# Three edits to one routed attention-MoE-FFN kernel: splits of the open expert's second matrix go from VectorE to GpSimd, early routing moves by a few steps, and the loads of the FFN weights and one scatter change their place

## The reference

```python
# attention: q, k, v are [4, 8, 768, 64]; 4 sink keys and a causal window of 128
scores = (q @ k.T) / sqrt(64), kept where key < 4 or 0 <= query - key < 128
a = softmax(scores); attn_out = a @ v
x = attn_out as [3072 tokens, 512]
# routed experts: top 1 of 8, D = 512, F = 1024
logits = x @ w_gate + modality_bias[modality_id]
e = argmax(logits); gate_w = softmax(logits)[e]
out[t] = gate_w * (relu(x[t] @ w1[e]) @ w2[e])
# FFN: 512 -> 2048 -> 512
h = out @ w_in; g = h * sigmoid(1.702 * h); result = g @ w_out
```

## Time and profile before

| | us |
|---|---|
| median of 3 runs | 1104.38 |
| profiled execution, time | 1103.77 |
| its span | 1102.0 |
| TensorE busy | 1090.4 |
| VectorE busy | 434.9 |
| ScalarE busy | 385.5 |
| GpSimd busy | 347.3 |

### The profile page before, as it was taken

The page is one execution under the profiler, slowest core; times in us unless marked ns, Lnnn a source line. Parts: engine busy times, 40 slices in busy tenths (PEclk is TensorE's granted clock), DMA queues, the critical chain, the costliest instruction groups (busy, mean ns, idle before and its releaser), DMA issues.

```text
span 1102.0 us, 18596 instructions
## 1 busy us (share of the span) xinstructions
PE 1090.4 (99%) x5883; PEld 932.3 (85%) x5884; DVE 434.9 (39%) x1112; ACT 385.5 (35%) x798; POOL 347.3 (32%) x484
## 2 busy tenths in 40 slices
PE   9999999999999999999999999999999999999998
PEld 9999999988888888888888888888888888888887
DVE  5666666679321234122364223222323222222222
ACT  3666667754222133222353222222222222222222
POOL 8899999852466212121120001001001001000100
PEclk9999999999999999999999999999999999999999
DMA  9998899415731133121041001001000001000101
GB/s 217 234 257 202 226 233 245 128 49 181 265 126 38 57 106 132 38 84 40 29 181 58 20 1 48 20 8 42 25 10 38 19 19 38 0 0 0 39 1 39
DMA packets 59700, 96.27 MB, mean 87 GB/s; under 512 B 8192, under 2 KB 33024, under 8 KB 59648
## 3 DMA queue, kind: packets, MB, share of 16 engines
q1 hardware_dynamic: 53888, 76.75, 25.0%
q0 software_dynamic: 5760, 18.89, 5.0%
HBM read 76.21 MB, written 19.41 MB: 87 GB/s over the span
## 4 chain that ended last, share of the span: by engine, by line
PE 94%; DVE 2%; issue 2%; ACT 2%; DVEq 0%; POOL 0%; ACTq 0%; POOLq 0%
PE psum L1264 8%; PE psum L1262 8%; PE psum L1263 8%; PE psum L1255 8%; PE psum L1254 8%; PE psum L1253 8%; PE psum L968 5%; PE psum L1193 4%; PE psum L1162 4%; PE psum L1199 4%; PE psum L1196 4%; PE psum L1166 4%; PE psum L1170 4%; PE psum L943 3%; PE psum L1181 2%; PE psum L931 2%
## 5 line engine op out<-in xcount | busy, mean ns | idle before, releaser
L2048 DVE TENSOR_TENSOR g<-psum,g 128x512 f32<-128x512 f32 x96 | 66.3, 691 | 292.2 <-ACT g L1483 292.2
L1483 ACT ACTIVATE g<-psum 128x512 f32<-128x512 f32 x96 | 57.3, 598 | 305.4 <-PE psum L1255 304.6
L1262 PE MATMUL psum<-w_hi,gT_hi 128*128 128x512 f32 x384 | 151.4, 394 | 0.0
L900 POOL DMA_INDIRECT out<-o_out,out_rows x20 | 21.5, 1074 | 409.3 <-ACT o_out L1503 404.7
L1264 PE MATMUL psum<-w_hi,gT_lo 128*128 128x512 f32 x384 | 149.6, 390 | 0.0
L1263 PE MATMUL psum<-w_lo,gT_hi 128*128 128x512 f32 x384 | 149.6, 390 | 0.0
L1255 PE MATMUL psum<-x2T,win_lo 128*128 (+1 forms) x384 | 149.6, 389 | 0.0
L1253 PE MATMUL psum<-x2T,win_hi 128*128 (+1 forms) x384 | 149.6, 389 | 0.0
L1254 PE MATMUL psum<-x2T,win_hi 128*128 (+1 forms) x384 | 149.4, 389 | 0.0
L968 PE MATMUL psum<-v_sb,pT 128*128 128x73 f32 x704 | 106.2, 270 | 3.2 <-DVE pT L1773 1.6
L1761 DVE CUSTOM_DVE_ANT_0 s_msk<-psum,mask_sb 128x260 f32<-128x260 f32 (+1 forms) x192 | 75.1, 403 | 68.8 <-PE psum L932 37.6
(11 more groups left out here) (313 smaller groups left out, 1884.9 us busy)
## 6 DMA issues: line engine op xcount, KB each, us to landing
qk_raw<-qkT SPq DMA_DIRECT2D x64, 384.0 KB, 7.5
stage<-w SPq DMA_DIRECT2D x12, 1024.0 KB, 7.0
x<-y_rows SPq DMA_DIRECT2D x24, 256.5 KB, 2.6
vT_sb<-vT SPq DMA_DIRECT2D x16, 384.0 KB, 5.1
v_sb<-vP SPq DMA_DIRECT2D x16, 384.0 KB
x_rows<-x_sb SPq DMA_DIRECT2D x16, 384.0 KB, 3.3
win_raw<-w SPq DMA_DIRECT2D x16, 256.0 KB, 4.3
win_raw<-w_in SPq DMA_DIRECT2D x16, 256.0 KB, 5.3
```

What stands on the lines that cost most here:

```text
L1262: pe.matmul(psum[:, OB[t], :], gh, hi, start=(f == 0), stop=False)
L2048: dve.tensor_tensor(g32[:, f % 2, :], psum[:, FB[f % 2], :], g32[:, f % 2, :], ALU.mult)\
```

## The change

- **Splits.** All 16 parts are subtracted by GpSimd: part j behind head 21 + j up to head 31 (11 parts), parts 11 to 13 behind the `pre_biased` add, parts 14 and 15 behind `tiles_seen`. VectorE's two subtractions of 128x2048 go, and with them the semaphore `open_low`.
- **Early routing.** `EXP_AT` goes from 38 to 41, the best from step 34 to 35, the lead from 37 to 38, `lower` from 31 to 37, the gates from 42 to 44, `whole_tiles` and `rows_in_tile` from 50 to 46. The two corrections of `rank_t` come from behind the attention to step 48. The logits of the last batch are added for 7 heads at once in step 49, not for 6 in step 44 and one more in step 49.
- **Tables.** `make_ends` stands inline ahead of `gather_i`.
- **Loads.** SyncE issues all 16 loads of `win_raw` behind `y_ready` 2.
- **Scatter.** `scatter_open(1)` and its landing come ahead of `gather(3)`, not behind it.

```diff
-    EXP_AT, RANK_AT_STEP = 38, 43
+    EXP_AT, RANK_AT_STEP = 41, 43
...
-            for half in range(2):
-                sp.wait_ge(y_ready, OPEN + half)
-                for n in range(half * 2 * PIECES, (half + 1) * 2 * PIECES):
-                    load_win(n)
+            sp.wait_ge(y_ready, OPEN)
+            for n in range(QUARTERS * PIECES):
+                load_win(n)
...
-                if OPEN_BACK <= h < OPEN_BACK + OPEN_PARTS // 2:
+                if h >= OPEN_BACK:
                     split_open(h - OPEN_BACK)
 
             pool.wait_ge(logits_added, B - 1)
             pool.tensor_tensor(lg[:, 0:PRE, :], lg[:, 0:PRE, :], bias_of[:, 0:PRE, :], ALU.add).then_inc(pre_biased, 1)
 
+            for j in range(B * H - OPEN_BACK, OPEN_PARTS - 2):
+                split_open(j)
             pool.wait_ge(best_found, 1)
...
             pool.sem_inc(tiles_seen, 1)
 
+            for j in range(OPEN_PARTS - 2, OPEN_PARTS):
+                split_open(j)
             pool.wait_ge(rows_known, 1)
...
             finish_scatter()
+            scatter_open(1)
+            end_open(1)
             pool.wait_ge(runs_ready, 1)
...
                 gather(t + 3)
-                if t == 0:
-                    scatter_open(1)
-                    end_open(1)
...
-                    pe.wait_ge(open_low, hf + 1)
+                    pe.wait_ge(open_split, 4 * (hf + 3))
...
-                if n == 34:
+                if n == 35:
                     dve.wait_ge(pre_biased, 1)
                     dve.tensor_reduce(best[:, pre], lg[:, pre, :], AX.X, ALU.max).then_inc(best_found, 1)
-                if n == 37:
+                if n == 38:
                     dve.wait_ge(ties_marked, 1)
                     dve.tensor_reduce(lead[:, pre], tied[:, pre, :], AX.X, ALU.max).then_inc(lead_found, 1)
-                if n == 31:
+                if n == 37:
                     then(dve.tensor_tensor(lower[:], e_col, e_row, ALU.is_gt))
-                if n == 42:
+                if n == 44:
                     make_gates(pre, 1)
...
-                if n == HT + 2:
+                if n == 46:
                     whole_tiles(pre)
                     rows_in_tile(pre).then_inc(rows_known, 1)
-                if n == 44:
-                    add_heads(B - 1, H - 2)
+                if n == HT:
+                    then(dve.tensor_scalar(own_rank[:, 0, 0:QT], rank_t[:, 0:QT], 0.0, -float(4 * SLOTS),
+                                           ALU.is_lt, ALU.mult))
+                    then(dve.tensor_tensor(rank_t[:, 0:QT], rank_t[:, 0:QT], own_rank[:, 0, 0:QT], ALU.add))
+                if n == HT + 1:
+                    add_heads(B - 1, H - 1)
                     add_biases(own)
-                if n == HT + 1:
-                    add_head(H - 2)
...
-            for q in range(2, QUARTERS):
-                dve.wait_ge(open_high, 4 * (q + 1))
-                dve.tensor_tensor(win_lo[:, q, :], win_raw[:, q, :], win_hi[:, q, :].bitcast(F32), ALU.subtract)\
-                   .then_inc(open_low, 1)
```

More of the change, by code:

```diff
@@ L366, in program @@
         open_expert_known, open_marked, open_inverted = (sem(f"open_{k}") for k in ("expert_known", "marked", "inverted"))
-        open_indexed, open_high, open_split, open_low = (sem(f"open_{k}") for k in ("indexed", "high", "split", "low"))
+        open_indexed, open_high, open_split = (sem(f"open_{k}") for k in ("indexed", "high", "split"))
         open_loaded = [sem(f"open_loaded{k}") for k in range(OPEN_PARTS // 2)]
@@ L1608, in add_biases, with add_last_head @@
                 then(dve.tensor_tensor(lg[:, tiles, :], lg[:, tiles, :], bias_of[:, tiles, :], ALU.add))
-            def add_head(h):
+            def add_last_head():
                 then(dve.tensor_tensor(lg[:, own, :], lg[:, own, :],
-                                       lg_parts[:, h, :].rearrange("p (t e) -> p t e", t=QT), ALU.add))
+                                       lg_parts[:, H - 1, :].rearrange("p (t e) -> p t e", t=QT), ALU.add))
             def find_best(tiles):
@@ L1853, in _ @@
             each_step(step)
-            add_head(H - 1)
+            add_last_head()
             find_best(own)
@@ L1863, in _ @@
             make_gates(own, 2)
-            then(dve.tensor_scalar(own_rank[:, 0, 0:QT], rank_t[:, 0:QT], 0.0, -float(4 * SLOTS),
-                                   ALU.is_lt, ALU.mult))
-            then(dve.tensor_tensor(rank_t[:, 0:QT], rank_t[:, 0:QT], own_rank[:, 0, 0:QT], ALU.add))
             count, tiles, tend = ranks_ps[:, QT, :], rank_t[:, NTILE:NTILE + E], e_cnt[:, 3, :]
@@ L1899, in _ @@
             hT_lows(0)
-            for q in range(2, QUARTERS):
-                dve.wait_ge(open_high, 4 * (q + 1))
-                dve.tensor_tensor(win_lo[:, q, :], win_raw[:, q, :], win_hi[:, q, :].bitcast(F32), ALU.subtract)\
-                   .then_inc(open_low, 1)
             busy, runs_before = e_cnt[:, 4, :], e_cnt[:, 5, :]
+            then(dve.tensor_tensor(tend, base_e[:], tiles, ALU.add))
+            then(dve.tensor_scalar(busy, tiles, 0.0, None, ALU.is_gt))
             tab = [P, SLOTS, E]
@@ L1908, in _ @@
             slot_col = col(iota_row[:, 0:SLOTS], tab)
[L1910 to L1916, removed]
+            then(dve.tensor_tensor(ends, slot_col, e_cnt[:, 3:4, :].broadcast_to(tab), ALU.is_ge))
+            then(dve.tensor_tensor(counted, ends, e_cnt[:, 4:5, :].broadcast_to(tab), ALU.mult))
+            then(dve.tensor_reduce(table_f[:, 0:SLOTS], counted, AX.X, ALU.add))
             dve.wait_ge(ohs_used, 1)
@@ L2006, in first_low @@
                    .then_inc(split, 1)
-            make_ends()
             make_flags()
```

## The result

The changed kernel took 1117.57 us (median; 1116.35 to 1119.84), the kernel before beside it 1105.38 (1103.77 to 1106.85): ratio 1.0113, 95% interval 1.0089 to 1.0137. It is slower, by 12.2 us between the medians where 8.3 were forecast, and 0.6 us above the range. The profiled execution of after took 1116.31 us with a span of 1114.5, 12.5 more than before's 1102.0.

A forecast was written before the change was run, and what follows sets the result against it. TensorE, busy 1090.4 of 1102.0 us, was taken as the bound, so only its idle time counts. 4.8 + 0.6 + 3.2 - 0.3 = +8.3 us gave 1112.7 us, range 1106.0 to 1117.0.

The forecast's parts named there:

- Ranking, +4.8: Early ranking, step 43, last batch: GpSimd's added splits delay `tiles_seen`, so it starts 4.8 us later (4.3 to 5.3).
- VectorE in steps 44 to 51, +0.6: Small operations moved ahead of the `pT_sinks` copy, which TensorE's last value products want: +0.6 us (0 to 1.0).
- VectorE after step 51, 0: Two subtractions leave VectorE, tables come earlier, but TensorE's own work hides this: 0, at most 0.25 us to win.
- Stall at `gather(3)`, +3.2: TensorE waits for `gather(3)`'s rows, queued behind the open tiles' scatter under the weight loads: +3.2 us (0 to 6.1).
- Next gather, -0.3: The 0.34 us wait ahead of L1053 at 307.10 goes, as that gather meets the traffic's end: -0.3 (0 to -0.6).
- The clock: in the sum 0, as a rival +1.8 with 0.26: Rival: idle between steps 42 and 43 drops TensorE to 1.2 GHz, losing 1.8 us behind it; 1114.5 us, chance 0.26.
- a loss of about 1 us for the scatter: By packet-by-packet turns, GpSimd's 256 KB transfers each land about 1 us late, without a `gather(3)` stall; prediction sided against it.

The follow-up runs named there:

- fill: Changed kernel plus 24 useless 128x128 matmuls at step 40 and 24 ahead of the ranking's wait; 1121.76 us, ratio 1.0155.
- splits_only: Kernel before with only the splits changed: all 16 parts on GpSimd, VectorE's two subtractions gone; 1110.09 us, ratio 1.0040.
- no_splits: Changed kernel with VectorE doing parts 8 to 15 again as in the kernel before; 1114.15 us, ratio 1.0079.
- late_three: Changed kernel with parts 11 to 13 moved from behind `pre_biased` to behind `tiles_seen`; 1114.92 us, ratio 1.0085.
- before_gather_late: Kernel before with GpSimd's gathers of the open tiles moved behind `tiles_seen`; 1103.89 us, ratio 0.9966.
- before_loads_together: Kernel before with all loads of the window's weights in one go behind the first open tile; 1106.86 us, ratio 0.9993.
- fill10: Changed kernel plus 10 useless 128x128 matmuls at step 40 and 10 ahead of the ranking's wait; 1117.72 us, ratio 1.0109.
- loads_halved: Changed kernel with SyncE's wait between the two halves of the `win_raw` loads put back; 1114.02 us, ratio 1.0071.
- scatter_back: Changed kernel with `scatter_open(1)` and its landing put back behind `gather(3)`; 1110.85 us, ratio 1.0044.

## Why the prediction was wrong, by its steps

- **Ranking, +4.8: right.** 4.70 in the profile, 4.96 counted from GpSimd's last split of a head, 4.89 from the splits alone. `below` at 224.46 for 224.8, `tiles_seen` 4.70 later, `lower` without cost ahead of the wait. The stand was expected in one piece of 5 us between steps 42 and 43. It came as 2.33 at step 40, where TensorE needs what VectorE copies in step 39 (`v_sb`, L1813), and that stands behind VectorE's wait of step 38, and 2.01 ahead of the ranking; in between TensorE worked at half clock.
- **VectorE in steps 44 to 51, +0.6: right.** 0.62 with the clock held up (fill); of this only 0.30 is seen as waiting in after, where the clock was low. The forecast was a choice between 0 and 1.0, so that it came to the hundredth is luck.
- **VectorE after step 51, 0: right.** The lag is the same at 253.47 and at 282.47.
- **Stall at `gather(3)`, +3.2: mis-sized; it measured 4.96.** The place, the owner and the cause hold, and the bounds (0 to 6.1) too. The scatter's hold was taken as 6.0, in the middle between 3.7 and 8.3 of the rows; it measured 8.0 in the terms of the sum (7.9 us to the landing; the 8.9 above hold 0.9 of the 1.9 that the sum has behind the landing). That is 2.0 of error; the scatter started 0.3 later than reckoned, the gather was taken as 6.5 and measured about 6.2, and TensorE asked 0.2 later. All GpSimd times there are 6.5 later by then, as are the loads. What failed is the idea that the scatter would meet only the middle of the traffic: the 16 loads ran to 291.87, not to 290.0 (the reckoned 283.5 in after's time), `stage` followed at 294.66, and the DMA share is 1.02 or more in every window from 290 to 306. So the scatter of 290.12 had the full traffic for all of its time.
- **Next gather, -0.3: right in sign.** -0.64.
- **The clock: in the sum 0, as a rival +1.8 with 0.26; it measured 1.17 + 1.73 = 2.9.** This is the step that failed, more than any other. The rival had the right mechanism and nearly the right price for one fall. That the price fits is in part luck: it was worked out from the warm-up, where the clock column reads 1.00, and the two falls differ from it and from each other in length. It had one fall; there were two, since the gather stall, a term of the sum, was never asked the question that was asked of the ranking. The argument against it, that TensorE partly waits behind the ranking anyway, does hold where the clock is back before a wait that GpSimd ends (splits_only), and not where it is not (after, no_splits, late_three).

Of the 4.2 us between the 8.3 of the sum and the 12.5 of the spans, the clock has 2.9 and the stall 1.8; the next gather gives 0.3 back. With the stall at 4.96 and the clock at 2.9 the sum is 4.7 + 0.6 + 5.0 - 0.6 + 2.9 = +12.6, against 12.5 in the spans.

The rule of the Trainium skill on the clock (TensorE: Matmul & The Clock Gate, Part 1), that an idle TensorE goes back to 1.2 GHz, agrees with the trace: 0.50 behind 2.33 and 4.80 us of idle time. It does not cover the fall behind `sort_tokens`, ahead of which the rows show TensorE busy. The rule of the Trainium skill on the turns that a DMA engine takes between its queues, packet by packet (DMA: Bandwidth & Descriptors, Queues, rings and completion order), by which the prediction estimated a loss of about 1 us for the scatter, is not enough for what was measured here: 7.9 us to the landing with the loads in one go, 3.4 with them in halves.

Two things stay open. The mean clock of separate executions says that falls come and go: before itself reads 1.000 in 10 and 0.995 to 0.999 in 31 of the 41 that ran beside the experiments, at a mean of 1105.2 us for the former and 1107.9 for the eleven at 0.997. A fall behind `sort_tokens` and nowhere else gives a mean of 0.998 (before_gather_late, before_loads_together). So part of what splits one run from the next, and some tenths of a per cent in the comparisons, may be this; no run separated it. And why it falls there in some executions and not in others was not settled.

## What to carry to other kernels

Where TensorE is 99% busy, ask of every stall in the sum, not only of the longest, whether the clock falls behind it; here one stood behind 2.33 us, and each fall that wasn't covered cost 1.2 to 1.7 us more. A fall costs nothing where the clock is back before a wait that another engine's chain ends (seen in splits_only). And it was work taken off GpSimd, which sets that wait, that gained 0.34% (before_gather_late), while matmuls put into the stand to hold the clock gained nothing (fill, fill10). And two edits that each cause no stall alone (an order on GpSimd's queue, a burst on SyncE's) are to be costed together, with the loaded durations of the rows and not with a mean of loaded and unloaded.

## What the runs showed of the hardware that was not expected

- The granted clock can fall with no stand of TensorE in the rows ahead of it. Behind 24 matmuls of 128x32 (`sort_tokens`) the windows read 0.55 and 0.60 (before_gather_late) and 0.72 and 0.70 (loads_halved), and the stretch to the next transposes took 9.7 us for 8.1. It did so in 8 of the 14 profiled executions, for 1.6 us each time, and not in those of before and after.
- The length of the stand alone does not say whether the clock falls. It fell behind stands of 1.73 us (fill10, to 0.57) and 2.02 us (no_splits, to 0.81 and 0.77 as means of 4 us), and stayed at 1.00 behind 1.67 us (before) and 1.66 us (before_loads_together); behind `sort_tokens` there was no stand.
- The indirect scatter of the second open tile took 3.5 us from the issue to the landing in before and 3.4 in loads_halved, with the loads in two halves, and 7.6 in scatter_back and 7.9 in after, with all 16 in one go and `stage` behind them. The DMA share over its time was 0.45 (before, 286 to 290) and 0.63 (loads_halved, 294 to 298), and 1.04 in the other two (293 to 301 and 290 to 298).
- Rows with the clock at 0.50 show 512-column matmuls at 2.07 us for four, against 1.07 to 1.19.
